# One token tile of 512 consecutive tokens instead of two halves of 256, and a sum-complete count for each output block

## What is computed

```
x  = attention(q, k, v, proj)          # (B*S, H*D) = (1536, 512)
h  = x @ w_in                          # (1536, 2048)
g  = h if h >= 1, 0 if h <= -1, else (h + 1)**2 / 4
x  = g @ w_out                         # (1536, 512)
h  = x @ w_in2 ;  g = h - tanh(h)
out = g @ w_out2
```

## Time and profile before

| | us |
|---|---|
| median of 3 runs | 797.55 (797.17 to 797.69) |
| the profiled execution | 796.39 |
| its span in the profile | 794.4 |
| PE busy | 765.7 (96%) |
| DVE busy | 422.4 (53%) |
| ACT busy | 355.0 (45%) |
| POOL busy | 326.3 (41%) |

### The profile page before, as it was taken

The page is one execution under the profiler, slowest core; times in us unless marked ns, Lnnn a source line. Parts: engine busy times, 40 slices in busy tenths (PEclk is TensorE's granted clock), DMA queues, the critical chain, the costliest instruction groups (busy, mean ns, idle before and its releaser), DMA issues.

```text
span 794.4 us, 11750 instructions
## 1 busy us (share of the span) xinstructions
PE 765.7 (96%) x3712; PEld 637.0 (80%) x3712; DVE 422.4 (53%) x757; ACT 355.0 (45%) x701; POOL 326.3 (41%) x267
## 2 busy tenths in 40 slices
PE   4999999999999999999999999999999999999997
PEld 2788888888888788878887888778888888888885
DVE  2999999999996665343334455541213222222222
ACT  2888889889885333333334323331212212222121
POOL 4789889899899993000000267760000000000000
PEclk8999999999999999999999999999999999999999
DMA  5533423433132332000000022210001000010001
GB/s 193 179 103 112 152 78 116 145 104 104 61 98 80 133 110 78 0 1 1 0 1 0 26 86 99 98 61 1 1 0 42 11 0 0 0 53 0 0 0 53
DMA packets 17864, 47.25 MB, mean 59 GB/s; under 512 B 2288, under 2 KB 4464, under 8 KB 17840
## 3 DMA queue, kind: packets, MB, share of 16 engines
q1 hardware_dynamic: 17840, 46.94, 18.4%
HBM read 38.87 MB, written 3.15 MB: 53 GB/s over the span
## 4 chain that ended last, share of the span: by engine, by line
PE 80%; POOL 5%; issue 5%; DVE 4%; ACT 3%; DMA 2%; SPq 1%; DVEq 0%; POOLq 0%; ACTq 0%
PE ps L489 33%; PE ps L564 30%; PE ps L466 5%; PE ps L480 5%; PE ps L452 2%; PE ps L455 2%; PE ps L423 2%; POOL probs L346 2%; POOL k_b L331 1%; ACT probs L610 1%; DMA k_raw<-kk 1%; DVE g_raw L805 1%; ACT g_hi L692 1%; DVE row_den L735 1%; POOL q_b L303 1%
## 5 line engine op out<-in xcount | busy, mean ns | idle before, releaser
L489 PE MATMUL ps<-x_hi,w 128*128 (+1 forms) x768 | 255.0, 396 | 0.0
L813 DVE TENSOR_TENSOR g_lo<-g_raw,g_hi 128x512 fp32r<-128x512 f32 x96 | 72.4, 754 | 268.5 <-ACT g_hi L692 268.5
L692 ACT ACTIVATE g_hi<-g_raw 128x512 fp32r<-128x512 f32 x96 | 60.8, 633 | 294.9 <-PE ps L564 266.3
L489 PEld LDWEIGHTS ps<-x_hi,w 128*128 128x128 f32 x768 | 144.4, 188 | 33.9
L489 PE MATMUL ps<-x_lo,w 128*128 (+1 forms) x384 | 152.1, 396 | 0.0
L564 PE MATMUL ps<-g_hi,w 128*128 128x512 f32 x384 | 125.6, 391 | 3.1 <-DVE g_lo L813 3.1
L564 PE MATMUL ps<-w,g_hi 128*128 128x512 f32 x384 | 118.6, 390 | 0.0
L303 POOL TENSOR_SCALAR w<-stage 128x1024 fp32r<-128x1024 f32 x32 | 38.1, 1191 | 165.4 <-PE ps L564 163.5
L743 DVE TENSOR_TENSOR p_lo<-ps,p_hi 128x384 fp32r<-128x384 f32 x192 | 97.8, 551 | 9.6 <-ACT p_hi L620 7.7
L346 POOL TENSOR_SCALAR probs<-probs,row_inv 128x768 f32<-128x768 f32 x96 | 86.9, 909 | 23.5 <-DVE row_inv L737 23.5
L620 ACT ACTIVATE p_hi<-ps 128x384 fp32r<-128x384 f32 x192 | 84.7, 489 | 24.3 <-PE ps L466 22.7
(11 more groups left out here) (48 smaller groups left out, 900.8 us busy)
## 6 DMA issues: line engine op xcount, KB each, us to landing
stage<-weights SPq DMA_DIRECT2D x32, 512.0 KB, 3.3
qk_raw<-qk SPq DMA_DIRECT2D x16, 384.0 KB, 3.5
q_raw<-qq SPq DMA_DIRECT2D x16, 384.0 KB, 3.2
k_raw<-kk SPq DMA_DIRECT2D x16, 384.0 KB, 3.8
q_a<-q_b SPq DMA_DIRECT2D x16, 192.0 KB
v_raw<-v SPq DMA_DIRECT2D x16, 192.0 KB, 2.4
out<-stage SPq DMA_DIRECT2D x12, 256.0 KB, 2.3
q_b<-bits SPq DMA_DIRECT2D x16, 54.0 KB
```

What stands on the lines that cost most here:

```text
L489: last = nc.tensor.matmul(ps[:, f % H_BANKS, :], w[:, f, wp, k * P:(k + 1) * P], xs[:, :, k, bass.ds(t * TOK, TOK)], start=(k == 0 and wp ...
L692: nc.scalar.activation(g_hi[:, slot, :], g_raw[:, slot, :], ACT.Copy).then_inc(g_hi_ready, 1)
L813: nc.vector.tensor_tensor(g_lo[:, slot, :], g_raw[:, slot, :], g_hi[:, slot, :].bitcast(F32), ALU.subtract).then_inc(g_split, 1)
```

## The change

The heads are handed over in another order: pair p now is chunk p // 2 of batch p % 2, so chunk 3 comes last for both batches, with batch 0 ahead of batch 1. x is stored as `[P, KC, B * S]`, and a token tile is 512 consecutive rows of the 1536: tile 0 lies in batch 0 alone, tile 1 in both, tile 2 in batch 1. The moving operand of `hidden_part` is one run of 512 columns. Tile 0 needs nothing of the last pair, so all 16 part products of the first four f are `early_hidden`, with their counts of `h_ready`, and the wait for the first half of the last pair is gone. A new semaphore `y_summed` is counted by the last product of each of the blocks m = 0, 1, 2 in project(15), and each copy of an output block waits for its own block; the block m = 3 still waits for `y_step`. Numbers of matmuls, of copies and of DMAs, their sizes, and the inputs' shapes stay.

```diff
-TOK = 256
-TT = S // TOK
+TOK = 512
+TT = B * S // TOK
...
-        x_hi = sb("x_hi", [P, B, KC, S], F32R)
-        x_lo = sb("x_lo", [P, B, KC, S], F32R)
+        x_hi = sb("x_hi", [P, KC, B * S], F32R)
+        x_lo = sb("x_lo", [P, KC, B * S], F32R)
...
+        def y_done(eng, tile, m):
+            if m < 3:
+                eng.wait_ge(y_summed, 3 * tile + m + 1)
+            else:
+                eng.wait_ge(y_step, G_SLOTS + FC * (tile + 1))
...
-                    row = (m // 2) * S + (m % 2) * P + t * TOK
+                    row = t * TOK + m * P
...
-                                            xs[:, :, k, bass.ds(t * TOK, TOK)],
+                                            xs[:, k, bass.ds(t * TOK, TOK)],
...
-                f, k = i // (KC - 1), i % (KC - 1)
+                f, k = i // KC, i % KC
...
-                hidden_part(0, f, k)
+                last = hidden_part(0, f, k)
+                if k == KC - 1:
+                    last.then_inc(h_ready, 1)
...
-            for i in range(PT_TILES - 1, HEAD * (KC - 1)):
+            for i in range(PT_TILES - 1, HEAD * KC):
                 early_hidden(i)
...
+                    if f == FC - 1 and m < 3:
+                        last.then_inc(y_summed, 1)
...
-            pe.wait_ge(x_last_ready, 1)
-            for f in range(HEAD):
-                hidden_part(0, f, KC - 1).then_inc(h_ready, 1)
             token_tile(0, 0)
             pe.wait_ge(x_last_ready, 2)
...
-                act.wait_ge(y_step, G_SLOTS + FC * (t + 1))
                 for m in range(4):
-                    nc.scalar.activation(x_hi[:, :, m, bass.ds(t * TOK, TOK)],
-                                         ps[:, 4 + m, :].rearrange("p (b s) -> p b s", b=B), ACT.Copy)\
+                    y_done(act, t, m)
+                    nc.scalar.activation(x_hi[:, m, bass.ds(t * TOK, TOK)], ps[:, 4 + m, :], ACT.Copy)\
                         .then_inc(y_hi_ready, 1)
...
-                act.wait_ge(y_step, G_SLOTS + FC * (TT + t + 1))
                 act.wait_ge(out_stored, 16 + 64 * t)
                 for m in (0, 2):
+                    y_done(act, TT + t, m)
                     nc.scalar.activation(stage[:, m // 2, 0:DM], ps[:, 4 + m, :], ACT.Copy).then_inc(out_copied[m], 1)
...
-                dve.wait_ge(y_step, G_SLOTS + FC * (TT + t + 1))
                 dve.wait_ge(out_stored, 16 + 64 * t)
                 for m in (1, 3):
+                    y_done(dve, TT + t, m)
                     nc.vector.tensor_copy(stage[:, m // 2, DM:2 * DM], ps[:, 4 + m, :]).then_inc(out_copied[m], 1)
```

More of the change, by code:

```diff
@@ L133, in build @@
         w = sb("w", [P, FC, 2, CH], F32R)
[L134 to L137, removed]
+        g_hi = sb("g_hi", [P, 2, TOK], F32R)
+        g_lo = sb("g_lo", [P, 2, TOK], F32R)
+        g_raw = sb("g_raw", [P, 2, TOK])
+        g_mid = sb("g_mid", [P, 2, TOK])
         ps = ctx.enter_context(nc.psum_tensor("ps", [P, 8, BANK], F32))
@@ L193, in build @@
         y_step = sem("y_step")
+        y_summed = sem("y_summed")
         y_hi_ready = sem("y_hi_ready")
@@ L208, in rows @@
             return p * S
-        x_hi_flat = x_hi[:, :, :, :].rearrange("p b c s -> p (b c s)")
-        x_lo_flat = x_lo[:, :, :, :].rearrange("p b c s -> p (b c s)")
+        def y_done(eng, tile, m):
[3 more added lines that the diff above has]
+                eng.wait_ge(y_step, G_SLOTS + FC * (tile + 1))
+        x_hi_flat = x_hi[:, :, :].rearrange("p c s -> p (c s)")
+        x_lo_flat = x_lo[:, :, :].rearrange("p c s -> p (c s)")
         @block.sync
@@ L820, in _ @@
                     dve.wait_ge(y_hi_ready, 4 * t + m + 1)
-                    nc.vector.tensor_tensor(x_lo[:, :, m, bass.ds(t * TOK, TOK)],
-                                            ps[:, 4 + m, :].rearrange("p (b s) -> p b s", b=B),
-                                            x_hi[:, :, m, bass.ds(t * TOK, TOK)].bitcast(F32), ALU.subtract)\
+                    nc.vector.tensor_tensor(x_lo[:, m, bass.ds(t * TOK, TOK)], ps[:, 4 + m, :],
+                                            x_hi[:, m, bass.ds(t * TOK, TOK)].bitcast(F32), ALU.subtract)\
                         .then_inc(y_free, 1)
@@ L863 @@
     mask_consts[:, 4 * HROWS:] = row_consts
-    qT = q.reshape(HEADS, S, D).transpose(0, 2, 1)
-    kT = k.reshape(HEADS, S, D).transpose(0, 2, 1)
+    order = [b * H + 2 * c + s for c in range(KC) for b in range(B) for s in range(2)]
+    qT = q.reshape(HEADS, S, D).transpose(0, 2, 1)[order]
+    kT = k.reshape(HEADS, S, D).transpose(0, 2, 1)[order]
     arrays = {
@@ L870 @@
         "qk": np.concatenate([qT, kT], axis=1),
-        "v": np.ascontiguousarray(v.reshape(HEADS, QT, P, D).transpose(0, 2, 1, 3)).reshape(HEADS, P, QT * D),
+        "v": np.ascontiguousarray(v.reshape(HEADS, QT, P, D).transpose(0, 2, 1, 3)[order]).reshape(HEADS, P, QT * D),
         "mask_consts": mask_consts,
```

## The result

| | before | after |
|---|---|---|
| median | 797.49 us (6 runs, 796.95 to 797.69) | 793.27 us (6 runs, 792.53 to 794.2) |
| profiled execution | 796.39 us | 793.87 us |
| its span | 794.4 us | 792.0 us |

The ratio is 0.9949, with a 95% interval from 0.9936 to 0.9961: 4.2 us faster. The forecast was 786.4 us, and its range began at 784.4 and ended at 791.0. The time lies outside, on the side of the rival "the two runs are free", which had 794.9 us and a chance of 0.10.

The account below looks back on a forecast made before the run. The prediction took PE, busy for 96% of the span, to bound the kernel. Hidden matmul pace 8.5 us, handover from attention 0.9 and tail 1.7 made 11.1 us off 797.55: 786.4 us, range 784.4 to 791.0.

Parts of the forecast that it names:

- the two runs are free: Rival: the hidden matmuls' extra 7.4 ns come from something x keeps, so only handover and tail gain; 794.9 us, chance 0.10.

## What to carry to other kernels

A difference in pace between two groups of matmuls in one trace names no cause, as long as the groups differ in more than one thing; before it is made a term of a sum, list the address of every operand beside its shape. Where a stream of fp32r matmuls reloads its weights each time, try the same start by 256 bytes for moving and stationary operand: here a pad of 416 bytes was worth 9.2 us by the trace, more than twice the change under study. (Only matmuls of 512 columns and the five distances of the table were run.) One profile gives only one draw of a wait: the wait ahead of the first projection was 0.70, 0.85 and 1.54 us in three.

## What the runs showed of the hardware

A 512-column fp32r matmul with a fresh 128 x 128 weight block started every 226.7 ns when the distance of the two operands in a partition was a multiple of 256 bytes (two kernels with a pad, one with x on top, weights as moving operand, the kernel before with a pad), and every 233.2 to 234.2 ns when it was 32, 96 or 128 bytes more than such a multiple. Neither the number of runs (1, 2, 4, 64), nor the PSUM bank, nor twelve sums in a row into one bank, nor zeros in the data changed that. Why a distance should matter no run shows. The Trainium skill, "SBUF — State Buffer", section "Who interferes with whom", gives TensorE two independent read ports, one for the moving operand and one for the weight loads, and says that it never waits on anyone. It speaks of waits between engines; taken for TensorE's own two reads as well, it would make no distance cost anything. The measurement decides: the distances of 32, 96 and 128 bytes cost 6.5 to 7.5 ns a matmul.
